# Eighteen operand distances in the second network's first layer: gaps between three weight matrices, each tile's x pieces at a place of its own

## The chip, the cores and the metric

The kernel runs on one core of one Trainium2 chip. The metric is device microseconds of one execution, the median of several; lower is better. Three runs are given for the kernel before. All times below are microseconds (us) unless marked ns.

## The reference

Attention with a decaying state runs over four sequences of 768 tokens, 8 heads of 48 channels. Its 3,072 x 384 result goes through a gated network and then through a second network, the only one that the change touches:

```python
def _moe_ref(x, w_gate, w_val, w_out, rms_g):
    ...
    g = xn @ w_gate
    silu = g * (1.0 / (1.0 + np.exp(-g)))
    val = xn @ w_val
    return (silu * val @ w_out).astype(np.float32)

def _moe2_ref(x, w1, w2, w3, w_out):
    h = np.maximum(np.maximum(x @ w1, x @ w2), x @ w3)
    return (h @ w_out).astype(np.float32)
```

All is float32. In the second network x is 3,072 x 384, w1, w2 and w3 are 384 x 768 and w_out is 768 x 384.

## The kernel before

The tokens are cut into six tiles of 512 (128 tokens of each of the four sequences). Attention of a tile runs interleaved with the gated network of the tile before; a last pass of the gated network runs alone; then the second network goes over the six tiles one after the other. Each engine has its own instruction stream, written out by hand, and the streams meet in semaphores: `after(engine, semaphore, tile, per_tile, nth)` waits for a count.

Every float32 product is made of three matmuls of a rounded type (`split_products`, the lines 484, 485 and 486 of the profile). Each operand is split into a rounded part, hi, and the rest, lo, and the three are hi x hi, hi x lo and lo x hi. In each, a 128 x 128 piece of weights is loaded into TensorE (a LDWEIGHTS record, engine "PEld") and then up to 512 columns of the other operand stream past it (a MATMUL record, engine "PE").

The first layer of the second network, in `phase2_tile` of the tensor block, takes for each of 6 column groups f and each of the matrices n = w1, w2, w3 three chunks c of 128 input channels: 6 x 3 x 3 x 3 = 162 matmuls of 512 columns. The weights stand, x streams. The results go to PSUM banks, ScalarE copies the first of three (line 840), VectorE takes the two maxima (lines 1115 and 1118), ScalarE and GpSimd split the result into hi and lo (lines 857 and 1236). The second layer is 4 x 6 x 3 = 72 matmuls of 384 columns, with the hidden values standing and `wo2` streaming.

x of a tile is loaded from scratch in DRAM to `xf` (the memory of `xn`), and then ScalarE (`split_x2_hi`, line 778) and VectorE (`split_x2_lo`, line 1034) split it into `x_hi` and `x_lo`, three chunks each. They do so for tile i + 1 when the last first-layer matmul of tile i is done, which is while TensorE runs the second layer of tile i. Before the change the buffers are `x_hi` and `x_lo`, which the first network uses too, at the start of the memory that the kernel allocates; `w123` lies behind the first network's weights:

```python
        x_hi = sb("x_hi", [P, KC, TOK], F32R)
        x_lo = sb("x_lo", [P, KC, TOK], F32R)
        xn = sb("xn", [P, B, DM])
        ...
        x1s = sb("x1s", [P, KC, TOK])
        act_h = sb("act_h", [P, 2, TOK])
        ...
        wg = [p1(f"wg_{s}", [P, KC, FF], F32R) for s in ("hi", "lo")]
        wv = [p1(f"wv_{s}", [P, KC, FF], F32R) for s in ("hi", "lo")]
        wo = [p1(f"wo_{s}", [P, FC, DM], F32R) for s in ("hi", "lo")]
        h_hi = p1("h_hi", [P, 2, TOK], F32R)
        h_lo = p1("h_lo", [P, 2, TOK], F32R)
```

P = 128, T = 128, TOK = 512, B = 4, DM = 384, KC = 3, FF = 1536, FC = 12, FF2 = 768, FC2 = 6, TILES = 6; an element has 4 bytes. Buffers are allocated one behind the other, and memory of a closed stage is given out again. On TensorE, tile 0 of the second network is written out and tiles 1 to 5 are a hardware loop (`pe.Fori`); on VectorE and ScalarE tiles 0 and 5 are written out and 1 to 4 are a loop.

Of the kernel before, what the change touches and what calls it, by code (L numbers as in the profile page):

```python
# [31 lines left out]
F32 = mybir.dt.float32  # L32
F32R = mybir.dt.float32r
BF16 = mybir.dt.bfloat16
U8 = mybir.dt.uint8
ACT = mybir.ActivationFunctionType
ALU = mybir.AluOpType
AX = mybir.AxisListType

P = 128  # L40
# [5 lines left out]
def rwkv_moe_kernel(nc, rc, kc, wc, r, k, v, u, g_w1, v_w1, o_w1, rms_g, w1, w2, w3, o_w2, out):  # L46
    B, TILES, _, _, PAIRS, _ = rc.shape
    S, H, D = r.shape[1:]
    DM, FF = g_w1.shape
    FF2 = w1.shape[1]  # L50
    TOK = B * T
    KC = DM // P
# [11 lines left out]
    with ExitStack() as ctx:  # L64
        def sb(name, shape, dt=F32, stack=ctx):
            return stack.enter_context(nc.sbuf_tensor(name, shape, dt))

        def psum(name, shape):
            return ctx.enter_context(nc.psum_tensor(name, shape, F32))

        def sem(name):
            return ctx.enter_context(nc.semaphore(name))
# [5 lines left out]
# [3 lines that stand above are left out]
        xf = xn[:, :, :].rearrange("p b n -> p (b n)").rearrange("p (c t) -> p c t", t=TOK)  # L81
# [36 lines left out]

        late = ExitStack()
        la = lambda name, shape, dt=F32: sb(name, shape, dt, late)  # L120
        w123 = [[la(f"w{i + 1}_{s}", [P, KC, FF2], F32R) for s in ("hi", "lo")] for i in range(3)]
        stage2 = la("stage2", [P, 2, FF2])
        late.close()
        phase1.close()
# [1 line left out]
        p2 = lambda name, shape, dt=F32: sb(name, shape, dt, phase2)  # L126
# [2 lines left out]
        h2_hi = p2("h2_hi", [P, FC2, TOK], F32R)  # L129
        h2_lo = p2("h2_lo", [P, FC2, TOK], F32R)  # L130
        ostage = p2("ostage", [P, 2, DM])
        phase2.close()

        ps_gate = psum("ps_gate", [P, TOK])
        ps_val = psum("ps_val", [P, TOK])
# [68 lines left out]
        x2_hi = sem("x2_hi")  # L204
        x2_lo = sem("x2_lo")
# [11 lines left out]
        def after(eng, s, tile, per_tile=1, nth=0):  # L217

            n = tile * per_tile + nth
            if not isinstance(n, int) or n > 0:  # L220
                eng.wait_ge(s, n)
# [257 lines left out]
        def _(pe):  # L479
            mm = nc.tensor.matmul  # L480

            def split_products(dst, lhs, rhs, start, stop):

                mm(dst, lhs[0], rhs[0], start=start, stop=False)  # L484
                mm(dst, lhs[0], rhs[1], start=False, stop=False)  # L485
                return mm(dst, lhs[1], rhs[0], start=False, stop=stop)  # L486
# [149 lines left out]
            def phase2_tile(i):  # L636
                for f in range(FC2):
                    cols = slice(f * P, (f + 1) * P)
                    for n in range(3):
                        if f == 0:  # L640
                            if isinstance(i, int) and i == 0:
                                pe.wait_ge(wt2_lo, (n + 1) * KC)
                        if isinstance(i, int) and i == 0 and f == 1 and n == 0:
                            pe.wait_ge(x1_copied, KC * PASSES)

                        after(pe, (m1_done, m2_done, m3_done)[n], i, FC2, f - 1)
                        for c in range(KC):
                            if f == 0 and n == 0:
                                after(pe, x2_lo, i, KC, c + 1)
                            wt = w123[n]  # L650
                            last = split_products(bank3[f % 2][n], (wt[0][:, c, cols], wt[1][:, c, cols]),
                                                  (x_hi[:, c, :], x_lo[:, c, :]), c == 0, c == KC - 1)
                        last.then_inc(mm3_done[n], 1)
                if isinstance(i, int) and i == 0:
                    pe.wait_ge(wt2_lo, len(pieces2))

                order = [(b, f) for b in range(B) for f in range(FC2)]
                order.remove((0, FC2 - 1))
                order.insert(FC2 - 1 + FC2 // 2, (0, FC2 - 1))
                for b, f in order:  # L660
                    if f == 0:
                        after(pe, out_copied, i, B, b - 1)
                    after(pe, h2_lo_done, i, FC2, f + 1)
                    toks = slice(b * T, (b + 1) * T)
                    last = split_products(bank_out[b % 2][:, 0:DM], (h2_hi[:, f, toks], h2_lo[:, f, toks]),
                                          (wo2[0][:, f, :], wo2[1][:, f, :]), f == 0, f == FC2 - 1)
                    if f == FC2 - 1:
                        last.then_inc(out_full, 1)


            pe.wait_ge(val_used, FC * PASSES)
            phase2_tile(0)
            with pe.Fori(1, TILES) as i:
                phase2_tile(i)


# [1 line left out]
        def _(act):  # L678
# [92 lines left out]
            def split_x2_hi(i):  # L771
                after(act, xf_in, i, 16, 16)
                if isinstance(i, int) and i == 0:
                    act.wait_ge(val_full, FC * PASSES)
                else:
                    after(act, mm3_done[2], i, FC2, 0)
                for c in range(KC):
                    nc.scalar.activation(x_hi[:, c, :], xf[:, c, :], ACT.Copy).then_inc(x2_hi, 1)

            def load_piece2(n):  # L780
                _, last = loads_before(n)
# [12 lines left out]
            def weight_piece2(n):  # L794
                act.wait_ge(st2_in[stage_of[n]], 16 * (loads_before(n)[0] + 1))
                nc.scalar.activation(pieces2[n][0], stages2[stage_of[n]], ACT.Copy).then_inc(wt2_hi, 1)
                for later in range(4, len(pieces2)):
                    if n == max(later - 3, loads_before(later)[1]):
                        load_piece2(later)
# [34 lines left out]
            def phase2_tile(i, last=False):  # L834
                if isinstance(i, int) and i == 0:
                    act.wait_ge(out_done, FC * PASSES)
                for f in range(FC2):
                    after(act, mm3_done[0], i, FC2, f + 1)
                    after(act, h2_lo_done, i, FC2, f - 1)
                    nc.scalar.activation(h2f[:, f % 2, :], bank3[f % 2][0], ACT.Copy).then_inc(m1_done, 1)  # L840
                    if f:
                        hidden_hi(i, f - 1)
                    if isinstance(i, int) and i == 0 and f % 2 == 0:
                        weight_piece2(EARLY2 + f // 2)
                hidden_hi(i, FC2 - 1)
                if not last:
                    split_x2_hi(i + 1)
                for b in range(B):
                    after(act, out_full, i, B, b + 1)
                    after(act, out_stored[b % 2], i, 16 * B // 2, 16 * (b // 2))  # L850
                    nc.scalar.activation(ostage[:, b % 2, :], bank_out[b % 2][:, 0:DM], ACT.Copy
                                         ).then_inc(out_copied, 1)

            def hidden_hi(i, f):
                after(act, m3_done, i, FC2, f + 1)
                after(act, out_full, i, B, 0)
                nc.scalar.activation(h2_hi[:, f, :], h2f[:, f % 2, :], ACT.Copy).then_inc(h2_hi_done, 1)  # L857

            phase2_tile(0)
            with act.Fori(1, TILES - 1) as i:  # L860
                phase2_tile(i)
            phase2_tile(TILES - 1, last=True)


        @block.vector
        def _(dve):
            tt = nc.vector.tensor_tensor
# [163 lines left out]
            def split_x2_lo(i):  # L1031
                for c in range(KC):
                    after(dve, x2_hi, i, KC, c + 1)
                    tt(x_lo[:, c, :], xf[:, c, :], x_hi[:, c, :].bitcast(F32), ALU.subtract).then_inc(x2_lo, 1)

            def x_split_lo(n):
                toks = tokens(n)[0]
# [72 lines left out]
            def phase2_tile(i, last=False):  # L1110
                for f in range(FC2):
                    dst = h2f[:, f % 2, :]
                    after(dve, m1_done, i, FC2, f + 1)
                    after(dve, mm3_done[1], i, FC2, f + 1)
                    tt(dst, dst, bank3[f % 2][1], ALU.max).then_inc(m2_done, 1)  # L1115
                    after(dve, m2_done, i, FC2, f + 1)
                    after(dve, mm3_done[2], i, FC2, f + 1)
                    tt(dst, dst, bank3[f % 2][2], ALU.max).then_inc(m3_done, 1)
                    if isinstance(i, int) and i == 0 and f % 2 == 0:
                        weight_piece2(EARLY2 + f // 2)  # L1120
                if not last:
                    split_x2_lo(i + 1)

            phase2_tile(0)
            with dve.Fori(1, TILES - 1) as i:
                phase2_tile(i)
            phase2_tile(TILES - 1, last=True)


        @block.gpsimd  # L1130
# [147 lines left out]
```

## Time and profile before

| | us |
|---|---|
| median of three runs | 1040.18 |
| lowest and highest | 1038.83, 1042.09 |
| the profiled execution | 1042.37 |
| its span, first to last instruction | 1040.6 |
| TensorE busy with matmuls in it | 997.7 |
| from the first matmul of the second network to the end | 298.55 |

A profile is one execution. An engine's busy time is the time in which it had at least one record running. Neighbouring matmuls overlap in the records: each has a duration of 0.33 to 0.40 us, while one starts every 0.17 to 0.24 us. So the pace is read from starts, not from durations. Starts are printed to 10 ns; a pace is therefore taken over many matmuls, from the first start to the last.

### The profile page before, as it was taken

To read this page: it belongs to the slowest core of one execution; us is meant where nothing else is said; L and a number is where in the kernel's file an instruction comes from. 1 tells how busy PE (TensorE), PEld (TensorE's weight loads), DVE (VectorE), ACT (ScalarE), POOL (GpSimd) and SP (SyncE) were. 2 spreads that over 40 slices of the span, in tenths; PEclk is the share of its full clock that TensorE was granted. 3 is DMA by queue.
4 is the path that set the end of the run, shared out by engine and by line. 5 is a ranking of instruction groups with operands and counts; after the bars stand their busy time and mean duration, and the time that the engine had idled before them with its cause. 6 is when DMAs were issued, how large, how long until landed. Compare 5 with 4: busy or idle time off the path is not lost.

```text
span 1040.6 us, 16737 instructions
## 1 busy us (share of the span) xinstructions
PE 997.7 (96%) x5680; PEld 882.3 (85%) x5680; DVE 623.3 (60%) x1047; ACT 246.2 (24%) x488; POOL 489.2 (47%) x540
## 2 busy tenths in 40 slices
PE   4778988899999999999999999999999999999998
PEld 4778988888888888888888888888888888888988
DVE  7878798988776877778776867444332212121221
ACT  2132312222123121222122212333322212121211
POOL 7656586857574757566674757212010201011111
PEclk9689999999999999999999999999999999999999
DMA  6533312212112120303021220201301010101000
GB/s 200 161 89 96 97 46 77 74 50 96 58 60 63 55 97 3 108 12 133 18 88 34 91 63 5 92 31 61 122 0 61 1 61 8 53 15 45 23 8 31
DMA packets 36221, 64.65 MB, mean 62 GB/s; under 512 B 4928, under 2 KB 22720, under 8 KB 36160
## 3 DMA queue, kind: packets, MB, share of 16 engines
q1 hardware_dynamic: 30288, 52.12, 15.2%
q10 hardware_dynamic: 5872, 11.80, 3.5%
q8 instruction: 28, 0.46, 0.2%
q14 instruction: 33, 0.27, 0.1%
HBM read 54.46 MB, written 9.44 MB: 61 GB/s over the span
## 4 chain that ended last, share of the span: by engine, by line
PE 84%; DVE 5%; POOL 5%; issue 3%; ACT 1%; DMA 0%; SPq 0%; ACTq 0%; POOLq 0%; DVEq 0%
PE ps_sc L503 10%; PE ps_acc L484 8%; PE ps_acc L486 8%; PE ps_acc L485 8%; PE ps_gate L484 6%; PE ps_gate L486 6%; PE ps_val L484 6%; PE ps_gate L485 6%; PE ps_val L486 5%; PE ps_val L485 5%; PE ps_desk L527 3%; PE ps_sc L486 2%; PE ps_sc L484 2%; PE ps_sc L485 2%; POOL kT L1168 2%
## 5 line engine op out<-in xcount | busy, mean ns | idle before, releaser
L503 PEld LDWEIGHTS ps_sc<-rB,kT 128*128 128x128 f32 x1152 | 155.8, 202 | 36.8 <-DVE rB L913 18.0
L503 PE MATMUL ps_sc<-rB,kT 128*128 128x128 f32 x1152 | 162.2, 288 | 25.8 <-DVE A L938 10.6
L1168 POOL TENSOR_TENSOR kT<-kT,wT 128x256 f32<-128x256 f32 x164 | 140.0, 853 | 83.9 <-PE ps_sc L503 56.4
L1236 POOL TENSOR_TENSOR h_lo<-h2f,h_hi 128x512 fp32r<-128x512 f32 x36 | 46.3, 1285 | 247.5 <-ACT h_hi L857 247.5
L1139 POOL TENSOR_TENSOR h_lo<-act_h,h_hi 128x512 fp32r<-128x512 f32 (+1 forms) x83 | 97.7, 1178 | 108.8 <-ACT h_hi L707 104.2
L1175 POOL TENSOR_TENSOR rB<-rB,wT 64x256 f32<-64x256 f32 x144 | 121.1, 841 | 11.3
L913 DVE TENSOR_TENSOR rB<-rB,wT 64x256 f32<-64x256 f32 x144 | 96.1, 672 | 30.4 <-PE ps_sc L503 23.7
L484 PE MATMUL ps_gate<-x_hi,wg_hi 128*128 128x512 f32 (+1 forms) x252 | 97.0, 385 | 8.9 <-DVE act_h L888 6.9
L707 ACT ACTIVATE h_hi<-act_h 128x512 fp32r<-128x512 f32 (+1 forms) x84 | 47.9, 571 | 230.4 <-DVE act_h L891 230.2
L938 DVE COPY_PREDICATED A<-mask,ps_sc 128x512 f32<-128x512 uint8 x120 | 98.9, 824 | 0.0
L484 PE MATMUL ps_acc<-h_hi,wo_hi 128*128 128x512 f32 (+1 forms) x252 | 95.7, 380 | 0.5 <-POOL h_lo L1139 0.3
L484 PE MATMUL ps_val<-x_hi,wv_hi 128*128 128x512 f32 (+1 forms) x252 | 96.2, 382 | 0.0
L703 ACT ACTIVATE act_h<-ps_gate 128x512 f32<-128x512 f32 (+1 forms) x84 | 45.1, 536 | 212.8 <-PE ps_gate L486 212.6
L486 PE MATMUL ps_gate<-x_hi,wg_lo 128*128 128x512 f32 (+1 forms) x252 | 91.8, 364 | 0.0
L486 PE MATMUL ps_val<-x_hi,wv_lo 128*128 128x512 f32 (+1 forms) x252 | 91.7, 364 | 0.0
L485 PE MATMUL ps_gate<-x_lo,wg_hi 128*128 128x512 f32 (+1 forms) x252 | 91.2, 362 | 0.0
L485 PE MATMUL ps_val<-x_lo,wv_hi 128*128 128x512 f32 (+1 forms) x252 | 91.1, 362 | 0.0
L925 DVE TENSOR_TENSOR wT<-wT 128x128 f32<-128x128 f32 (+6 forms) x160 | 77.1, 490 | 23.4 <-POOL rB L1175 21.5
L486 PE MATMUL ps_acc<-h_hi,wo_lo 128*128 128x512 f32 (+1 forms) x252 | 90.9, 361 | 0.0
L485 PE MATMUL ps_acc<-h_lo,wo_hi 128*128 128x512 f32 (+1 forms) x252 | 90.5, 359 | 0.0
L1115 DVE TENSOR_TENSOR h2f<-h2f,ps_val 128x512 f32<-128x512 f32 x18 | 12.4, 688 | 106.2 <-PE ps_val L486 106.2
L891 DVE TENSOR_TENSOR act_h<-act_h,ps_val 128x512 f32<-128x512 f32 (+1 forms) x84 | 51.4, 612 | 35.4 <-PE ps_val L486 34.1
(136 smaller groups left out, 2028.7 us busy)
## 6 DMA issues: line engine op xcount, KB each, us to landing
kT<-in_k_channels SPq DMA_DIRECT2D x24, 256.0 KB, 3.4
wT<-in_w_channels SPq DMA_DIRECT2D x24, 256.0 KB, 4.0
rB<-in_r_channels SPq DMA_DIRECT2D x48, 128.0 KB, 2.6
kL<-in_k_tokens SPq DMA_DIRECT2D x24, 192.0 KB, 2.4
rL<-in_r_tokens SPq DMA_DIRECT2D x24, 192.0 KB, 2.5
vL<-in_v_tokens SPq DMA_DIRECT2D x24, 192.0 KB, 2.4
x_scratch<-x1s SPq DMA_DIRECT2D x6, 768.0 KB, 4.4
xn<-x_scratch SPq DMA_DIRECT2D x6, 768.0 KB, 4.3
```

The costliest lines, as they stand in the source:

```text
L484: mm(dst, lhs[0], rhs[0], start=start, stop=False)
L485: mm(dst, lhs[0], rhs[1], start=False, stop=False)
L486: return mm(dst, lhs[1], rhs[0], start=False, stop=stop)
L503: last = mm(ps_sc[:, j, q * T:(q + 1) * T], kT[2 * duo + j][:, q, :], rights, start=True, stop=True)
L707: nc.scalar.activation(h_hi[:, f % 2, toks], act_h[:, f % 2, toks], ACT.Copy).then_inc(h_hi_done, 1)
L891: tt(hidden, hidden, ps_val[:, toks], ALU.mult).then_inc(val_used, 1)
L913: tt(new, old, block_decay(2 * duo + j, 1 << level, 0, HEAD_ROWS[0]), ALU.mult).then_inc(r_even_scaled, 1)
L925: tt(left, left, half(w[:, :, :], h, 1)[:, :, 0:1], ALU.mult).then_inc(tot_done, 1)
L938: nc.vector.copy_predicated(dst, every_head.broadcast_to([P, H, n, h]), src.rearrange("p (g n h) -> p g n h", g=H, h=h)).then_inc(scores_u ...
L1139: tt(h_lo[:, f % 2, toks], act_h[:, f % 2, toks], h_hi[:, f % 2, toks].bitcast(F32), ALU.subtract).then_inc(h_lo_done, 1)
L1168: tt(half(kT[b][:, :, :], h, 0), half(kT[b][:, :, :], h, 0), block_decay(b, h, 1), ALU.mult).then_inc(k_scaled, 1)
L1175: tt(new, old, block_decay(b, h, 0, HEAD_ROWS[1]), ALU.mult).then_inc(r_odd_scaled, 1)
```

## The change

Three things are changed. Between w1 and w2, and between w2 and w3, unused gaps of 16 and 32 elements (64 and 128 bytes) are allocated. The split x of the second network no longer goes to `x_hi` and `x_lo` but to four new rooms (hi and lo, for even and for odd tiles), which lie in memory that the first network's weights no longer need, and in its room each tile's x starts at an offset of its own, `X2_AT`, counted in elements: 0, 4, 8, 12, 2, 6. As these offsets are numbers of the program, the loops over the second network's tiles on TensorE, ScalarE and VectorE are written out. GpSimd's and SyncE's streams stay as they are, and no semaphore count changes.

```diff
@@ -118,7 +118,11 @@
-        w123 = [[la(f"w{i + 1}_{s}", [P, KC, FF2], F32R) for s in ("hi", "lo")] for i in range(3)]
+        w123 = []
+        for i, gap in enumerate((0, 16, 32)):
+            if gap:
+                la(f"gap{i}", [P, gap])
+            w123.append([la(f"w{i + 1}_{s}", [P, KC, FF2], F32R) for s in ("hi", "lo")])
@@ -129,7 +133,15 @@
         ostage = p2("ostage", [P, 2, DM])
+        x2_room = [[p2(f"x2_{s}{i}", [P, KC * TOK + P], F32R) for s in ("hi", "lo")] for i in range(2)]
         phase2.close()
+
+        X2_AT = (0, 4, 8, 12, 2, 6)
+
+        def x2_piece(i, lo):
+
+            room = x2_room[i % 2][lo]
+            return room[:, X2_AT[i]:X2_AT[i] + KC * TOK].rearrange("p (c t) -> p c t", t=TOK)
...
@@ -649,9 +661,9 @@
                             wt = w123[n]
                             last = split_products(bank3[f % 2][n], (wt[0][:, c, cols], wt[1][:, c, cols]),
-                                                  (x_hi[:, c, :], x_lo[:, c, :]), c == 0, c == KC - 1)
+                                                  (x2_piece(i, 0)[:, c, :], x2_piece(i, 1)[:, c, :]), c == 0, c == KC - 1)
                         last.then_inc(mm3_done[n], 1)
...
@@ -669,8 +681,7 @@
             pe.wait_ge(val_used, FC * PASSES)
-            phase2_tile(0)
-            with pe.Fori(1, TILES) as i:
+            for i in range(TILES):
                 phase2_tile(i)
@@ -775,7 +786,7 @@
                 for c in range(KC):
-                    nc.scalar.activation(x_hi[:, c, :], xf[:, c, :], ACT.Copy).then_inc(x2_hi, 1)
+                    nc.scalar.activation(x2_piece(i, 0)[:, c, :], xf[:, c, :], ACT.Copy).then_inc(x2_hi, 1)
@@ -1031,7 +1040,7 @@
                     after(dve, x2_hi, i, KC, c + 1)
-                    tt(x_lo[:, c, :], xf[:, c, :], x_hi[:, c, :].bitcast(F32), ALU.subtract).then_inc(x2_lo, 1)
+                    tt(x2_piece(i, 1)[:, c, :], xf[:, c, :], x2_piece(i, 0)[:, c, :].bitcast(F32), ALU.subtract).then_inc(x2_lo, 1)
@@ -1121,10 +1130,8 @@
-            phase2_tile(0)
-            with dve.Fori(1, TILES - 1) as i:
-                phase2_tile(i)
-            phase2_tile(TILES - 1, last=True)
+            for i in range(TILES):
+                phase2_tile(i, last=i == TILES - 1)
```

The same is done to ScalarE's loop, and some tests of the tile number are shortened.

In the rows below, `x2_hi1` is the hi room of the odd tiles. First TensorE's stream where tile 0 of the second network ends and tile 1 begins, before:

```order
L484 MATMUL ps_desk<-wo2_hi,h2_hi 128x384
L485 MATMUL ps_desk<-wo2_lo,h2_hi 128x384
L486 MATMUL ps_desk<-wo2_hi,h2_lo 128x384
L673 UNCONDITIONAL_BRANCH
L673 ISA
L221 ISA
L484 MATMUL ps_gate<-x_hi,w1_hi 128x512
L485 MATMUL ps_gate<-x_lo,w1_hi 128x512
L486 MATMUL ps_gate<-x_hi,w1_lo 128x512
L221 REGISTER_ALU
L484 MATMUL ps_gate<-x_hi,w1_hi 128x512
```

And after, at the same place:

```order
L496 MATMUL ps_desk<-wo2_hi,h2_hi 128x384
L497 MATMUL ps_desk<-wo2_lo,h2_hi 128x384
L498 MATMUL ps_desk<-wo2_hi,h2_lo 128x384
L496 MATMUL ps_gate<-x2_hi1,w1_hi 128x512
L497 MATMUL ps_gate<-x2_lo1,w1_hi 128x512
L498 MATMUL ps_gate<-x2_hi1,w1_lo 128x512
```

The matmuls stand in the same order; the branch and the register instructions between them are gone, and x comes from another buffer. VectorE's stream at the end of tile 1, inside its loop, before:

```order
L1115 TENSOR_TENSOR h2f<-h2f,ps_acc 128x512
L1118 TENSOR_TENSOR h2f<-h2f,ps_acc 128x512
L221 ISA
L1034 TENSOR_TENSOR x_lo<-xn,x_hi 128x512
L221 REGISTER_ALU
L1034 TENSOR_TENSOR x_lo<-xn,x_hi 128x512
```

And after, at the end of tile 1:

```order
L1124 TENSOR_TENSOR h2f<-h2f,ps_acc 128x512
L1127 TENSOR_TENSOR h2f<-h2f,ps_acc 128x512
L1043 TENSOR_TENSOR x2_lo0<-xn,x2_hi0 128x512 x3
```

The three subtractions that make lo stay where they were, behind the tile's last maximum, and write to the even tiles' room.

## Rows read from the trace of the kernel before

**Rows 1.** the page: span, and each engine's busy time, share, instructions.
```profile
span 1040.6 us, 16737 instructions
PE 997.7 (96%) x5680; PEld 882.3 (85%) x5680; DVE 623.3 (60%) x1047; ACT 246.2 (24%) x488; POOL 489.2 (47%) x540
```

**Rows 2.** the page, the chain that ended last, by engine.
```profile
PE 84%; DVE 5%; POOL 5%; issue 3%; ACT 1%; DMA 0%; SPq 0%; ACTq 0%; POOLq 0%; DVEq 0%
```

**Rows 3.** windows, the second network's tiles 0, 1 and 4.
```profile
core 0: us, PE busy (x) PEld busy (x) DVE busy (x) ACT busy (x) POOL busy (x), PEclk, DMA share, GB/s
742.05:791.28 49.23, 49.23 (x235) 42.91 (x234) 13.44 (x18) 13.63 (x24) 7.74 (x6) 1.00 0.15 53
791.28:840.55 49.27, 49.27 (x236) 42.91 (x235) 10.83 (x15) 10.35 (x19) 7.71 (x6) 1.00 0.09 33
939.08:988.35 49.27, 49.27 (x236) 42.91 (x235) 10.83 (x15) 10.35 (x19) 7.71 (x6) 1.00 0.10 32
```

**Rows 4.** timeline, TensorE's matmuls, tile 0: start, duration in us.
```profile
742.05 0.39 PE L484 MATMUL ps_gate<-x_hi,w_hi 128*128 128x512 f32 x1
744.10 0.39 PE L484 MATMUL ps_val<-x_hi,w_hi 128*128 128x512 f32 x1
...
778.55 0.39 PE L486 MATMUL ps_acc<-x_hi,w_lo 128*128 128x512 f32 x1
```

**Rows 5.** timeline, TensorE's matmuls, second layer of tile 0.
```profile
785.74 0.33 PE L485 MATMUL ps_sc<-wo_lo,h_hi 128*128 128x384 f32 x1
...
791.11 0.33 PE L486 MATMUL ps_desk<-wo_hi,h_lo 128*128 128x384 f32 x1
```

**Rows 6.** timeline, TensorE's weight loads, start of tile 0.
```profile
742.05 0.19 PEld L485 LDWEIGHTS ps_gate<-x_lo,w_hi 128*128 128x128 f32 x1
742.29 0.19 PEld L486 LDWEIGHTS ps_gate<-x_hi,w_lo 128*128 128x128 f32 x1
```

**Rows 7.** timeline, TensorE's matmuls, start of tile 1.
```profile
791.28 0.39 PE L484 MATMUL ps_gate<-x_hi,w_hi 128*128 128x512 f32 x1
791.51 0.40 PE L485 MATMUL ps_gate<-x_lo,w_hi 128*128 128x512 f32 x1
791.74 0.40 PE L486 MATMUL ps_gate<-x_hi,w_lo 128*128 128x512 f32 x1
791.98 0.39 PE L484 MATMUL ps_gate<-x_hi,w_hi 128*128 128x512 f32 x1
...
793.36 0.39 PE L484 MATMUL ps_val<-x_hi,w_hi 128*128 128x512 f32 x1
```

**Rows 8.** groups by line, attention's matmuls, 98 to 660 us.
```profile
L503 PE MATMUL ps_sc<-rB,kT 128*128 128x128 f32 x984 | 129.8, 275 | 7.6 <-DVE A L938 6.0 <-issue 1.2 <-POOL rB L1175 0.3
L527 PE MATMUL ps_desk<-vL,A 128*128 128x48 f32 x352 | 42.0, 272 | 0.0
L522 PE MATMUL ps_desk<-state,rD 128*128 128x96 f32 x160 | 21.0, 274 | 0.1
```

**Rows 9.** timeline, attention scores of level 1, then of level 2.
```profile
175.95 1.07 PE L503 MATMUL ps_sc<-rB,kT 128*128 128x128 f32 x8
...
226.68 1.05 PE L503 MATMUL ps_sc<-rB,kT 128*128 128x128 f32 x8
```

**Rows 10.** the page, DMA queues: packets, MB, share of 16 engines.
```profile
q8 instruction: 28, 0.46, 0.2%
```

**Rows 11.** timeline, ScalarE's and VectorE's x pieces, tiles 0 and 1.
```profile
738.99 1.66 ACT L778 ACTIVATE x_hi<-xn 128x512 fp32r<-128x512 f32 x3
739.73 1.89 DVE L1034 TENSOR_TENSOR x_lo<-xn,x_hi 128x512 fp32r<-128x512 f32 x3
...
780.30 1.66 ACT L778 ACTIVATE x_hi<-xn 128x512 fp32r<-128x512 f32 x3
780.95 2.57 DVE L1034 TENSOR_TENSOR x_lo<-xn,x_hi 128x512 fp32r<-128x512 f32 x3 [1.22 <-ACT x_hi L778]
```

More of the change, by code:

```diff
@@ L640, in phase2_tile @@
                         if f == 0:
-                            if isinstance(i, int) and i == 0:
+                            if i == 0:
                                 pe.wait_ge(wt2_lo, (n + 1) * KC)
-                        if isinstance(i, int) and i == 0 and f == 1 and n == 0:
+                        if i == 0 and f == 1 and n == 0:
                             pe.wait_ge(x1_copied, KC * PASSES)
@@ L651, in phase2_tile @@
                             last = split_products(bank3[f % 2][n], (wt[0][:, c, cols], wt[1][:, c, cols]),
-                                                  (x_hi[:, c, :], x_lo[:, c, :]), c == 0, c == KC - 1)
+                                                  (x2_piece(i, 0)[:, c, :], x2_piece(i, 1)[:, c, :]), c == 0, c == KC - 1)
                         last.then_inc(mm3_done[n], 1)
-                if isinstance(i, int) and i == 0:
+                if i == 0:
                     pe.wait_ge(wt2_lo, len(pieces2))
@@ L857, in hidden_hi @@
                 nc.scalar.activation(h2_hi[:, f, :], h2f[:, f % 2, :], ACT.Copy).then_inc(h2_hi_done, 1)
-            phase2_tile(0)
-            with act.Fori(1, TILES - 1) as i:
-                phase2_tile(i)
-            phase2_tile(TILES - 1, last=True)
+            for i in range(TILES):
+                phase2_tile(i, last=i == TILES - 1)
         @block.vector
@@ L1122, in phase2_tile @@
                     split_x2_lo(i + 1)
-            phase2_tile(0)
-            with dve.Fori(1, TILES - 1) as i:
-                phase2_tile(i)
-            phase2_tile(TILES - 1, last=True)
+            for i in range(TILES):
+                phase2_tile(i, last=i == TILES - 1)
         @block.gpsimd
```

## The prediction

> **What bounds the kernel now.** I read the page first: the span and how much of it TensorE computes [rows 1]. TensorE is busy 96% of the span, and the chain that ended last is 84% TensorE [rows 2]. So a term counts if it changes the pace of the matmuls or makes them wait. The change touches only the second network, so I then cut that part into its six tiles (three of them in [rows 3]). The reader is to see that in each of the first five tiles TensorE is busy for the whole 49.23 to 49.27 us, that the clock is at its upper level (1.00, 2.4 GHz), and that VectorE, ScalarE and GpSimd are busy for 7.7 to 13.6 us of it. Nothing there waits for data; only the number of matmuls and their pace count.
>
> The pace stands in the timeline. In tile 0 the first layer has 162 matmuls of 512 columns. The first starts at 742.05, the last at 778.55 [rows 4], so 161 gaps take 36.50 us: 226.7 ns each. In the second layer, 384 columns, the rows at 785.74 and 791.11 are 31 gaps apart [rows 5]: 173.2 ns each. The two paces differ by 53.5 ns for 128 columns, 0.418 ns a column. 512 columns at that rate take 214 ns, so about 13 ns of each gap are not columns. Those 13 ns are the only thing here that a change of addresses could win: 972 first-layer matmuls (162 in each of 6 tiles).
>
> What can addresses do to them? The weight load of the next matmul starts with the current one [rows 4, 6]: the matmul at 742.05 streams x while the load at 742.05, 0.19 us long, reads the next 128 columns of weights. Both read SBUF at the same time. How far apart they read follows from the declarations. From x_hi to w1_hi lie four buffers of 6,144 bytes per partition, act_h with 4,096, six weight matrices of 18,432 and two h buffers of 4,096: 147,456 bytes, 288 times 512. Each further matrix is 9,216 bytes (18 times 512), each x chunk 2,048, each c step of the weights 3,072, each f step 512. So before the change every first-layer pair is at a distance that is a whole multiple of 512 bytes.
>
> **The change part by part.**
> Distances. The gaps shift w2 by 64 bytes and w3 by 64 + 128 = 192. The x pieces shift by 0, 16, 32, 48, 8 and 24 bytes, tile by tile. Modulo 256 this gives 6 x 3 = 18 different distances, and only tile 0 with w1 (54 matmuls) keeps the old one; 918 matmuls move. No row shows a first-layer matmul at another distance. From both sides: at best the 13.3 ns vanish, 918 x 13.3 ns = 12.2 us. At worst every gap is as long as the longest that the trace has between unstalled 512-column matmuls, 0.24 us at the start of tile 1 [rows 7]: 13.3 ns more, 12.2 us the other way. I take zero, for two reasons. Distances already differ between c, f, hi and lo by several multiples of 512, and the gap does not move. And both streams walk: the 128 weight columns are 512 bytes, x is 2,048 bytes in one matmul, so if both take their columns evenly over their records' time the distance between the two reading points sweeps through hundreds of bytes within each matmul. A shift of the start by 8 to 192 bytes then only changes where the sweep begins. The attention stage is weak support: moving operands whose starts step by 192 bytes (vL for A) and 384 bytes (state for rD) have records of 272 and 274 ns, against 275 ns for rB, which is always on the 512-byte grid [rows 8]. Weak, since these are short matmuls of two operand shapes and the weight load paces them.
>
> What speaks against zero: the gap isn't a constant of the operation. The first nine matmuls of tile 1 take 791.28 to 793.36, 2.08 us, those of tile 0 742.05 to 744.10, 2.05 us [rows 4, 7], and the first three gaps in tile 1 are 0.23, 0.23 and 0.24 us where the steady ones are 0.2267. The operands and distances are the same in both tiles; so a stall of some nanoseconds inside a matmul depends on how the two streams stand in time. That is why I keep over four in ten for a real effect.
>
> The Trainium skill, page "TensorE: Matmul & The Clock Gate", section "Part 2: What happens when you issue a matmul", says that TensorE has two independent SBUF read ports and that loading the next weights takes nothing from the running matmul. By this rule the change is worth exactly zero. The same page (section "Wait — 56ns, not 53.3ns?") gives 215.7 ns for 512 columns; the trace has 226.7, so 11 ns of each gap are something that the page does not have. An estimate from that page: if the new distances removed them, 918 x 11 = 10.1 us.
>
> Starts inside a 16-byte group. Tiles 4 and 5 start at 8 and 24 bytes. The nearest row is attention level 1, where rB is read in runs of two values, 8 bytes: eight records take 1.07 us, with longer runs 1.05 [rows 9]: 2.5 ns for 128 columns. Four times that, 10 ns, for 324 matmuls is 3.2 us. That is an upper bound, since a contiguous row only adds a partial group at its start; I take zero.
>
> Unrolled loops. TensorE, ScalarE and VectorE lose a branch and register arithmetic at each tile. TensorE pays 2.08 against 2.05 us at a tile start: 0.03 us x 5 = 0.15 us, if the loop is the reason and not the step from 384 to 512 columns; I take 0.15. The longer program must be fetched: instruction queue 8 takes 0.2% of the DMA engines' time now [rows 10], and tile 0, which is written out straight already, runs 49.23 us against 49.27 in the loop [rows 3]. Zero.
>
> ScalarE's and VectorE's x pieces. They write as many values as before, to other places, and no wait moves: the next tile's x is still split only after all first-layer matmuls of this one, so two rooms bring no earlier start. Their cover: in tile 0 ScalarE splits from 780.30 and VectorE ends at 780.95 + 2.57 = 783.52 [rows 11]; the next tile needs it at 791.28, 7.8 us later. At the border between the networks the cover is thin: VectorE's three pieces run from 739.73 to 741.62, the first is needed at 742.05 and the third some 1.4 us later [rows 4, 11]. Pieces twice as long would end at 743.51, and the first (0.63 us now) would be ready at 740.99: at most 0.1 to 0.2 us of waiting, once. What is queued behind them on VectorE is tile 0's first maximum, which is due only after 18 matmuls of the tile, 4.1 us past 742.05. Zero.
>
> Sum: -0.15 us on a span of 1040.6. The profiled execution took 1042.37 us, the median of the three runs is 1040.18; I put the difference on the median: 1040.0.
>
> **The rivals.**
> 1. The distance has no effect (above): 1040.0, own range 1038.5 to 1041.5. For it: the constant gap over all multiples of 512, the walking streams. Against it: the gaps that vary by nanoseconds. Chance 0.56.
> 2. Faster: equal remainders are the bad case, because the weight read and the x read meet in the same place of SBUF, and other distances part them. For it: 13 ns per matmul, whether 384 or 512 columns stream, which is what a fixed number of meetings with a fixed 128-column load would cost. All shifted pairs free: 1040.0 - 12.2 = 1028. More likely some distances help and others don't: half gives 6.1 us, 1034. Chance 0.24.
> 3. Slower: the old remainder is the good case, and a shifted pair stalls all the time as at the start of tile 1. There nine gaps average 231.1 ns, 4.4 more: 918 x 4.4 ns = 4.1 us, 1044. It decides from 3.4 ns per shifted matmul (3.1 us, 0.3%); bound 1052. Against it: nothing marks the old place as special. Chance 0.13.
> 4. Slower: the starts at 8 and 24 bytes cost 10 ns each, in tiles 4 and 5 alone: 3.2 us, 1043. Against it: a row has one partial group in 128. Chance 0.07.
>
> **How the numbers follow.** A difference of 0.3%, 3.1 us, is about what a measurement of this kernel can tell from no change. Same: case 1, 0.56. Faster: case 2, 0.24. Slower: cases 3 and 4, 0.20. The predicted time is case 1's. The range runs from 1033, case 2 with half of its bound and a little more, to 1046, cases 3 and 4 with their own sizes and some more. It leaves out case 2 near its full bound (about 0.10) and case 3 near its bound (about 0.06).
>
> **What would show it.** Right: in the changed profile all six tiles take 49.2 us, and the first layer's gap is 226.7 ns in each tile and for each matrix. Case 2 or 3 would show as 18 different paces, by tile and by matrix, with tile 0 and w1 at 226.7. Case 4 would show as tiles 4 and 5 longer by 1.6 us each, tiles 1 to 3 unchanged. VectorE's split in the changed tiles longer than 2.57 us would show that writes at odd places cost, hidden. The prediction is wrong if any steady gap is not 226.7.

## The result, and the profile after

The change makes the kernel slower: 1046.20 us against 1040.87, medians of six runs each, ratio 1.0054 (95% interval 1.0041 to 1.0068). I had forecast 1040.0 and a range from 1033 to 1046.

The page and the timeline of the changed kernel, span and engines first, then the first matmul of the second network's tiles 1 to 5, the first of tile 2's second layer (877.88) and the last of all (start, duration in us):

```profile
span 1044.2 us, 16568 instructions
PE 999.0 (96%) x5680; PEld 879.3 (84%) x5680; DVE 622.8 (60%) x1047; ACT 246.2 (24%) x488; POOL 490.4 (47%) x540
...
790.09 0.39 PE L496 MATMUL ps_gate<-x_hi,w_hi 128*128 128x512 f32 x1
...
840.09 0.39 PE L496 MATMUL ps_gate<-x_hi,w_hi 128*128 128x512 f32 x1
...
877.88 0.33 PE L496 MATMUL ps_sc<-wo_hi,h_hi 128*128 128x384 f32 x1
...
890.38 0.39 PE L496 MATMUL ps_gate<-x_hi,w_hi 128*128 128x512 f32 x1
...
940.66 0.39 PE L496 MATMUL ps_gate<-x_hi,w_hi 128*128 128x512 f32 x1
...
990.87 0.39 PE L496 MATMUL ps_gate<-x_hi,w_hi 128*128 128x512 f32 x1
...
1040.96 0.34 PE L498 MATMUL ps_desk<-wo_hi,h_lo 128*128 128x384 f32 x1
```

The second network begins at 740.33 (next fence) and ends with the span at 1044.2: 303.87 us, against 298.55 before, 5.3 more. That is as much as the medians differ (5.33). The two profiled spans differ by less, 3.6 us, because this execution reached the second network 1.7 us earlier (740.33 against 742.05; in all the traces of this case it is 739.4 to 744.7); the change touches nothing in the part before but where w2 and w3 lie. TensorE is still never idle in the second network up to its last matmul, and the granted clock there is 1.00, as before. The tiles take 49.76, 50.00, 50.29, 50.28 and 50.21 us, where [rows 3] has 49.23 to 49.27. So each tile is longer, tile 0 least.

The same number of matmuls runs at another pace. The nine-matmul groups of tile 0, first the one of w1, then w2, w3 and w1 again (timeline, the first matmul of each group):

```profile
740.33 0.39 PE L496 MATMUL ps_gate<-x_hi,w_hi 128*128 128x512 f32 x1
...
742.37 0.40 PE L496 MATMUL ps_val<-x_hi,w_hi 128*128 128x512 f32 x1
...
744.47 0.39 PE L496 MATMUL ps_sc<-x_hi,w_hi 128*128 128x512 f32 x1
...
746.53 0.39 PE L496 MATMUL ps_acc<-x_hi,w_hi 128*128 128x512 f32 x1
...
748.59 0.40 PE L496 MATMUL ps_acc<-x_hi,w_hi 128*128 128x512 f32 x1
```

w1, the only one at the old distance, takes 2.04 us for nine, as before. w2 (-64 bytes) takes 2.10, w3 (-192) 2.06: 233 and 229 ns each for 226.7. w1 after w3 takes 2.06 too (2.05 in the later groups), so a group at the old distance does not start at its old pace right away. Tile 2, whose x is 32 bytes on, has no group at the old pace: from 840.09 to its second layer at 877.88 are 162 matmuls in 37.79 us, 233.3 ns each. Over the six tiles the first layer has 5.35 us more (225.87 against 220.52), 5.8 ns for each of the 918 moved matmuls. Averaged over its six groups, each of the eighteen pairs of tile and matrix lies between 227.6 ns (tile 0, w1) and 234.6 ns (tile 3, w2). The second layer, whose operands kept their distances, takes 12.3 us as before.

VectorE's split, for which I had left a margin, did not change (timeline, x_lo for tile 1; [rows 11] has 2.57 too):

```profile
779.78 2.57 DVE L1043 TENSOR_TENSOR x_lo<-xn,x_hi 128x512 fp32r<-128x512 f32 x3 [1.22 <-ACT x_hi L789]
```

### The profile page after: what moved, and what is told of

Same layout as the page of the kernel before. It is cut to its first block, busy times and chain, and to the rows that moved or that the text cites. A ratio compares the mean times of both kernels' runs of the same rounds, so it can differ in the third digit from the quotient of the medians.

```text
span 1044.2 us, 16568 instructions
## 1 busy us (share of the span) xinstructions
PE 999.0 (96%) x5680; PEld 879.3 (84%) x5680; DVE 622.8 (60%) x1047; ACT 246.2 (24%) x488; POOL 490.4 (47%) x540
## 4 chain that ended last, share of the span: by engine, by line
PE 83%; DVE 6%; POOL 5%; issue 3%; ACT 1%; DMA 0%; SPq 0%; ACTq 0%; POOLq 0%; DVEq 0%
PE ps_sc L515 9%; PE ps_acc L496 8%; PE ps_acc L498 8%; PE ps_acc L497 8%; PE ps_gate L496 6%; PE ps_gate L498 6%; PE ps_val L496 5%; PE ps_gate L497 5%; PE ps_val L498 5%; PE ps_val L497 5%; PE ps_desk L539 3%; PE ps_sc L497 2%; PE ps_sc L498 2%; PE ps_sc L496 2%; POOL kT L1175 2%
## 5 line engine op out<-in xcount | busy, mean ns | idle before, releaser
L515 PE MATMUL ps_sc<-rB,kT 128*128 128x128 f32 x1152 | 159.7, 285 | 27.2 <-POOL rB L1182 12.9
L515 PEld LDWEIGHTS ps_sc<-rB,kT 128*128 128x128 f32 x1152 | 153.5, 199 | 38.1 <-DVE rB L922 19.4
L718 ACT ACTIVATE h_hi<-act_h 128x512 fp32r<-128x512 f32 (+1 forms) x84 | 47.9, 571 | 229.0 <-DVE act_h L900 228.8
```

Of the source, the lines that this page charges most:

```text
L515: last = mm(ps_sc[:, j, q * T:(q + 1) * T], kT[2 * duo + j][:, q, :], rights, start=True, stop=True)
L718: nc.scalar.activation(h_hi[:, f % 2, toks], act_h[:, f % 2, toks], ACT.Copy).then_inc(h_hi_done, 1)
```

## The experiments

Distance below is the remainder of (address of x less address of the weights) modulo 256 bytes. Paces are first start to first start of the next stretch over the number of matmuls. All experiments are variants of the changed kernel or of the one before; ratios are against the kernel before on the same chip, with the 95% interval in brackets, and the us behind a ratio are its distance from 1 times the median of before.

### Undo the distances, keep the rest

```diff
-        for i, gap in enumerate((0, 16, 32)):
+        for i, gap in enumerate((0, 0, 0)):
-        X2_AT = (0, 4, 8, 12, 2, 6)
+        X2_AT = (0, 0, 0, 0, 0, 0)
```

> The changed kernel with both kinds of offsets at zero: no gaps between the matrices, every tile's x at the start of its room. The new rooms and the written-out tiles stay. If the distances cost the time, all six tiles are back at 49.2 us and the median lies at that of before, within 1 us. If the rooms or the written-out loops cost it, the tiles stay at 49.8 to 50.3 us and the time 5 us above before.

Ratio 1.0001 (0.9988 to 1.0014). The first matmuls of tiles 0, 1, 2 and of tile 1's second matrix (timeline):

```profile
741.03 0.39 PE L496 MATMUL ps_gate<-x_hi,w_hi 128*128 128x512 f32 x1
...
790.26 0.39 PE L496 MATMUL ps_gate<-x_hi,w_hi 128*128 128x512 f32 x1
...
792.34 0.39 PE L496 MATMUL ps_val<-x_hi,w_hi 128*128 128x512 f32 x1
...
839.52 0.39 PE L496 MATMUL ps_gate<-x_hi,w_hi 128*128 128x512 f32 x1
```

Tiles of 49.23 and 49.26 us: the new rooms and the written-out loops cost nothing. They gain nothing either. Tile 1's first nine matmuls still take 2.08 us (790.26 to 792.34) though there is no loop any more, so my 0.15 us for the branches was wrong. That the slower start comes from the step from 384 to 512 columns, the other cause that I had named, is not shown either: in a run below one tile is entered from 384 columns without it, and one has it without such a step.

### The gaps alone, and the x offsets alone

The two halves of the change, each with the other set to zero as above.

> The gaps alone (w2 64 bytes on, w3 192), x of all tiles at the start of its room. By distances every tile is as tile 0 of the changed kernel: w1 about 227.6 ns, w2 232.9, w3 229.6 a matmul, first layer 37.27 us, a tile 49.75: 6 x 0.52 = 3.1 us over before. If only x's offsets mattered: as before.

> The x offsets alone, no gaps: in a tile all three matrices are at the same distance (0, 16, 32, 48, 8, 24 bytes). If the distance itself costs, w1, w2 and w3 of a tile all have w1's pace in the changed kernel (about 231.4, 234.1, 233.5, 232.4, 233.8 ns in tiles 1 to 5): some 5 us over before. If a change of distance from one matrix to the next costs, and a constant one settles, tiles 1 to 5 run at 226.7 ns and the time is that of before.

Gaps alone: ratio 1.0027 (1.0014 to 1.0040), 2.8 us. Offsets alone: 1.0048 (1.0031 to 1.0066), 5.0 us. Tiles 1 and 2 with the gaps alone, then with the offsets alone tiles 0 to 4 and tile 4's first matmul of 384 columns (timeline, first matmuls):

```profile
789.73 0.39 PE L496 MATMUL ps_gate<-x_hi,w_hi 128*128 128x512 f32 x1
...
839.52 0.39 PE L496 MATMUL ps_gate<-x_hi,w_hi 128*128 128x512 f32 x1
```

```profile
740.24 0.39 PE L496 MATMUL ps_gate<-x_hi,w_hi 128*128 128x512 f32 x1
...
789.46 0.39 PE L496 MATMUL ps_gate<-x_hi,w_hi 128*128 128x512 f32 x1
...
839.47 0.39 PE L496 MATMUL ps_gate<-x_hi,w_hi 128*128 128x512 f32 x1
...
889.75 0.39 PE L496 MATMUL ps_gate<-x_hi,w_hi 128*128 128x512 f32 x1
...
940.03 0.39 PE L496 MATMUL ps_gate<-x_hi,w_hi 128*128 128x512 f32 x1
...
977.82 0.34 PE L496 MATMUL ps_sc<-wo_hi,h_hi 128*128 128x384 f32 x1
```

With the gaps alone tile 1 takes 49.79 us, and so do tiles 2 to 4 (tile 0, 49.75). With the offsets alone tile 0 is back at 49.22 us, and tiles 1 and 2 take 50.01 and 50.28; in tile 4 the 162 matmuls run from 940.03 to 977.82, 233.3 ns each. There all three matrices are at one distance, 8 bytes, for 162 matmuls on end and the pace does not recover. So it is the distance that costs, not a change of distance. The two halves do not add up to the whole (2.8 + 5.0 against 5.3), as the combined distances are others, and none that is made of both shifts costs the sum of the two: the slowest, tile 3 with w2, is 7.9 ns over 226.7, where its halves are 6.6 and 6.2.

### Both operands moved together, and larger distances

```diff
-        for i, gap in enumerate((0, 16, 32)):
+        for i, gap in enumerate((16, 0, 0)):
-        X2_AT = (0, 4, 8, 12, 2, 6)
+        X2_AT = (16, 0, 32, 80, 112, 48)
```

> A gap of 64 bytes ahead of w1 and none later; x of the six tiles 64, 0, 128, 320, 448 and 192 bytes into its room. So tile 0 has both operands 64 bytes on, at distance 0; tiles 1 to 5 have x less w at -64, +64, +256, +384 and +128 bytes, the same for all three matrices. By distance tile 0 runs at 226.7 ns and tile 1 near 232.9 (w2 of tile 0 in the changed kernel). If an operand's own address counts, tile 0 is slower. If only changes of distance count, all are at 226.7. A multiple of 256 bytes may be as good as 0; then tile 3 is at 226.7.

Ratio 1.0027 (1.0014 to 1.0040). First matmul and first second-layer matmul (384 columns) of tiles 0, 1, 2 and 3; in tiles 0 and 3 also the tenth matmul (`ps_val`):

```profile
741.92 0.39 PE L496 MATMUL ps_gate<-x_hi,w_hi 128*128 128x512 f32 x1
...
743.99 0.39 PE L496 MATMUL ps_val<-x_hi,w_hi 128*128 128x512 f32 x1
...
778.68 0.34 PE L496 MATMUL ps_sc<-wo_hi,h_hi 128*128 128x384 f32 x1
...
791.18 0.39 PE L496 MATMUL ps_gate<-x_hi,w_hi 128*128 128x512 f32 x1
...
828.99 0.34 PE L496 MATMUL ps_sc<-wo_hi,h_hi 128*128 128x384 f32 x1
...
841.49 0.40 PE L496 MATMUL ps_gate<-x_hi,w_hi 128*128 128x512 f32 x1
...
878.58 0.33 PE L496 MATMUL ps_sc<-wo_hi,h_hi 128*128 128x384 f32 x1
...
891.07 0.39 PE L496 MATMUL ps_gate<-x_hi,w_hi 128*128 128x512 f32 x1
...
893.11 0.39 PE L496 MATMUL ps_val<-x_hi,w_hi 128*128 128x512 f32 x1
...
927.78 0.34 PE L496 MATMUL ps_sc<-wo_hi,h_hi 128*128 128x384 f32 x1
```

| tile | distance, bytes | first layer, us | a matmul, ns |
|---|---|---|---|
| 0 | 0, both 64 on | 36.8 | 226.9 |
| 1 | -64 | 37.8 | 233.3 |
| 2 | +64 | 37.1 | 229.0 |
| 3 | +256 | 36.7 | 226.7 |
| 4, 5 | +128 | 37.6 | 232.4 |

Moving both operands by 64 bytes leaves the steady pace as it was (the 0.2 ns of tile 0 are its first nine matmuls), moving one does not, and 256 bytes are as good as zero. (Tiles 4 and 5 had +384 and +128, the same modulo 256, and ran at the same pace.) The sign matters: +64 costs 2.2 ns, -64 costs 6.7.

The same trace speaks on the slow start. Tile 3 is entered from the 384-column layer, and its first nine matmuls take 2.04 us. Tile 0 is entered from the first network's 512-column matmuls and takes 2.07. So neither the loop nor the step in columns is the whole of it, and what sets the start of a tile stays open.

### Six more distances, and the second layer

X offsets of 1, 36, 40, 44, 63 and 62 elements, no gaps between the matrices, and

```diff
+        p2("gap_h2", [P, 16])
         h2f = p2("h2f", [P, 2, TOK])
         ...
+        p2("gap_back", [P, 48])
```

> Six more distances, the same for the three matrices of a tile: x is 4, 144, 160, 176, 252 and 248 bytes on (modulo 256: 4, -112, -96, -80, -4, -8). No theory says which of them is good; so far 0 and 256 give 226.7 ns and all others 228.9 to 234.1. If only the multiples of 256 are good, none is at 226.7 or under. Also, the hidden values h2, which stand in the second layer, lie 64 bytes on, so that wo2 less h2 is -64 bytes there: if the law holds at 384 columns too, that layer's gap goes from 173.3 to 180.0 ns (as 226.7 goes to 233.3), 6 x 72 x 6.7 ns = 2.9 us in all; if it is special to the first layer, it stays at 173.3.

Ratio 1.0087 (1.0065 to 1.0108), the slowest of all. The first layers take 38.47, 37.79, 37.94, 37.79, 37.20 and 37.78 us: 237.5 ns a matmul at +4 bytes, 233.3 at 144, 176 and 248, 234.2 at 160, 229.6 at 252. With those above, fourteen distances other than 0 have had a tile of their own, and all are slower than 0. The second layer surprised (first and last of its 72 matmuls, tiles 0 and 1):

```profile
779.90 0.34 PE L498 MATMUL ps_sc<-wo_hi,h_hi 128*128 128x384 f32 x1
...
792.20 0.34 PE L500 MATMUL ps_desk<-wo_hi,h_lo 128*128 128x384 f32 x1
...
830.17 0.34 PE L498 MATMUL ps_sc<-wo_hi,h_hi 128*128 128x384 f32 x1
...
842.71 0.33 PE L500 MATMUL ps_desk<-wo_hi,h_lo 128*128 128x384 f32 x1
```

71 gaps take 12.30 us in tile 0 and 12.54 in tile 1: 173.3 and 176.7 ns, at one and the same distance. Tiles 3 and 5 are at 176.7 too, tiles 2 and 4 at 174.7. The three tiles at 176.7 are those whose first layer ran at 233.3 ns; they are also the three odd ones. The last pair of experiments below asks which of the two it is.

### Which two reads must agree

```diff
+            hi = la(f"w{i + 1}_hi", [P, KC, FF2], F32R)
+            la(f"gap{i}_lo", [P, 16])
+            lo = la(f"w{i + 1}_lo", [P, KC, FF2], F32R)
+            w123.append([hi, lo])
+            la(f"gap{i}_back", [P, 48])
-        X2_AT = (0, 4, 8, 12, 2, 6)
+        X2_AT = ((0, 16), (0, 0), (16, 16), (16, 0), (0, 4), (0, 32))
```

Each pair is the offset of x_hi and of x_lo in a tile, in elements.

> Which two reads count. All three w_lo lie 64 bytes on, w_hi on the old place; x_hi and x_lo have offsets of their own. In tile 0 x_lo is 64 bytes on and x_hi is not. Then every matmul streams x from the same remainder as the weights that are loaded meanwhile for the next matmul, but in the second and third matmul of each three x and its own weights differ by 64. If the load that overlaps is what counts, tile 0 runs at 226.7 ns; if a matmul's own weights count, it is at 229 or more. Tile 1 has both x at 0: the load of w_lo overlaps x_lo at -64, one in three. Tile 2 has both x 64 on: two of three at +64. Tile 3 has x_hi alone 64 on: +64, -64, +64. Tile 4: 0, -48, 0; tile 5: 0, +64, 0.

One run, 1045.65 us. Tile 0, first matmul and first of its second layer:

```profile
741.64 0.39 PE L498 MATMUL ps_gate<-x_hi,w_hi 128*128 128x512 f32 x1
...
779.07 0.34 PE L498 MATMUL ps_sc<-wo_hi,h_hi 128*128 128x384 f32 x1
```

37.43 us, 231.0 ns. My idea that only the stream and the load beside it must agree gives 226.7 and falls. The other idea, a matmul's own weights, asked for 229 or more and is not refuted by this tile, but the prices of the table don't add up by it either: 0, +64 and -64 would average 229.6. Tiles 1, 3, 4 and 5, whose distances have no pattern in common, are all at 231.1 or 231.2; tile 2 is at 229.1. The counterpart leaves all weights alone (the gaps are zero) and moves x_lo only, but for tile 5:

```diff
-        X2_AT = (0, 4, 8, 12, 2, 6)
+        X2_AT = ((0, 64), (0, 16), (0, 32), (0, 48), (0, 4), (16, 32))
```

> All weights at the old place, x_hi at 0 in tiles 0 to 4, x_lo on by 256, 64, 128, 192 and 16 bytes; in tile 5 x_hi 64 and x_lo 128. If each pair of a stream and the load beside it has its own price and these add up, one in three pays: tile 0 226.7 ns, tile 1 226.7 + 2.2/3 = 227.4, tile 3 226.7 + 6.7/3 = 228.9, tile 2 about 228.6, tile 4 about 228.4. If what costs is that neighbouring streams start at different remainders, all of tiles 1 to 4 are near 231.1 ns, as four tiles of the run with w_lo 64 bytes on were, and tile 0 at 226.7.

One run, 1044.68 us. Tiles 2 and 3, first matmul and first of the second layer:

```profile
840.04 0.39 PE L496 MATMUL ps_gate<-x_hi,w_hi 128*128 128x512 f32 x1
...
877.84 0.34 PE L496 MATMUL ps_sc<-wo_hi,h_hi 128*128 128x384 f32 x1
...
890.35 0.39 PE L496 MATMUL ps_gate<-x_hi,w_hi 128*128 128x512 f32 x1
...
927.42 0.33 PE L496 MATMUL ps_sc<-wo_hi,h_hi 128*128 128x384 f32 x1
```

x_lo on by 256 (tile 0): 226.7 ns. By 192 (tile 3): 37.07 us, 228.9 ns, which is what adding up one -64 in three gives. By 64 (tile 1) 231.9, by 128 (tile 2) 233.3, by 16 (tile 4) 232.0: neither of the two theories. (Tile 5, x_hi on by 64 and x_lo by 128, is at 231.2.) So prices of single pairs don't add up, and a change from one stream to the next does not have one price. Which pairs of reads disturb each other stays open.

### Fewer weight columns

```diff
-        for i, gap in enumerate((0, 16, 32)):
+        for i, gap in enumerate((0, 0, 0)):
+        W_COLS = (128, 96, 64, 32, 128, 64)
-        X2_AT = (0, 4, 8, 12, 2, 6)
+        X2_AT = (0, 0, 0, 0, 48, 48)
-                    cols = slice(f * P, (f + 1) * P)
+                    cols = slice(f * P, f * P + W_COLS[i])
```

> What the 13.3 ns over the 213.3 ns of 512 columns are. Tiles 0 to 3 have distance 0 and load 128, 96, 64 and 32 weight columns a matmul (the other hidden channels of these tiles are left out); tiles 4 and 5 have distance -64 and load 128 and 64. If each group of weight columns read takes a slot from the stream of x, the excess falls with the columns: 226.7, about 223, 220, 217 ns; and at distance -64 from 233.3 to about 223 for 64 columns. If it is a fixed price of a change of weights, all of tiles 0 to 3 stay at 226.7 and tiles 4 and 5 at 233.3.

One run, 1048.75 us. Tile 3 (32 columns): a weight load, then first matmul and first of the second layer:

```profile
899.96 0.11 PEld L499 LDWEIGHTS ps_acc<-x_hi,w_lo 128*32 128x32 f32 x1
```

```profile
893.47 0.40 PE L497 MATMUL ps_gate<-x_hi,w_hi 128*32 128x512 f32 x1
...
931.00 0.34 PE L497 MATMUL ps_sc<-wo_hi,h_hi 128*128 128x384 f32 x1
```

The loads are shorter, 0.11 us for 0.19, and the matmuls are not: 37.53 us, 231.7 ns each; 230.0 with 96 and with 64 columns; at distance -64 232.7 with 64 columns for 233.3. Both theories fall, the second only by 3 to 5 ns at distance 0. The 13 ns are no price per weight column, and they are no constant: at distance 0 a full load of 128 columns is the best of the four.

### The first network and attention

In the kernel before, 64 bytes ahead of the gate weights (and 192 ahead of the output weights, which keep their remainder):

```diff
+        p1("gap_g", [P, 16])
         wg = [p1(f"wg_{s}", [P, KC, FF], F32R) for s in ("hi", "lo")]
         wv = [p1(f"wv_{s}", [P, KC, FF], F32R) for s in ("hi", "lo")]
+        p1("gap_back", [P, 48])
```

> The kernel before, with the first network's gate and value weights 64 bytes on (the output weights and all behind them on the old remainder), so x less weights is -64 bytes in 1512 matmuls of the first network. Nothing else is changed. If the law of the second network's first layer holds here, they take 233.3 ns each for 226.7: 10.1 us in all, of which the last pass (216 of them, nothing beside them) must show 1.4 us, and the interleaved passes most of theirs, since TensorE is busy over 90% there: +6 to +10 us. If the effect is special to the second network, the time stays.

Ratio 1.0054 (1.0035 to 1.0073), 5.6 us. A gate group, a value group and an output group of nine in the last pass (first matmul of each and of the next):

```profile
690.93 0.40 PE L486 MATMUL ps_gate<-x_hi,wg_hi 128*128 128x512 f32 x1
...
693.04 0.39 PE L486 MATMUL ps_val<-x_hi,wv_hi 128*128 128x512 f32 x1
...
695.13 0.39 PE L486 MATMUL ps_acc<-h_hi,wo_hi 128*128 128x512 f32 x1
...
697.20 0.40 PE L486 MATMUL ps_gate<-x_hi,wg_hi 128*128 128x512 f32 x1
```

Gate and value groups take 2.10 and 2.09 us, 233 ns a matmul, as in the second network. The output group, whose operands are at distance 0, takes 2.07 us: it begins slow and recovers in its course. From the last of attention's score matmuls (648.1 in both) to the second network are 95.5 us against 93.9: +1.6, where I expected 1.4. The price of -64 bytes is the same in another stage. Of the interleaved passes I expected up to 8.7 us more; the ratio leaves about 4 for them, give or take 2. Where the two profiled executions reach the end of these passes doesn't tell (the last score matmul stands at 648.1 in both, and at 645.5 in the attention experiment below), but the pace in them does. Over some 700 gaps under 0.26 us behind a gate or value matmul the mean is 229.8 ns in the trace of before and 233.2 here. So these matmuls, which attention's keep interrupting, were 3 ns slower than 226.7 to begin with and had only 3.4 ns to lose, half of my 6.7.

The same in attention, whose matmuls have 128 columns (a fourth gap behind the last kT brings the rest back):

```diff
+            if b:
+                at_(f"gap_k{b}", [P, 16])
             kT.append(at_(f"kT{b}", [P, PAIRS, T]))
```

> The kernel before, with the four kT buffers of attention 0, 64, 128 and 192 bytes on (64-byte gaps between them), so rB less kT is 0, -64, -128 and -192 bytes for the four sequences. These matmuls have 128 columns, and the weight load paces them (111 ns a record). If only a stream of x that is longer than the load is slowed by distance, the pace stays 111 ns for all four and the time is that of before. If the two reads disturb each other whatever the sizes, the sequences 1 to 3 are slower, by up to 6.7 ns a record; 3/4 of 1152 records, at most 5.8 us. A distance that is better than 0 here would make the kernel faster.

Ratio 0.9990 (0.9976 to 1.0004): the same. The group of these matmuls between 95 and 650 us (count | busy, mean ns of one) has records of 275 ns, as in [rows 8]:

```profile
L508 PE MATMUL ps_sc<-rB,kT 128*128 128x128 f32 x984 | 129.8, 275 | 7.7 <-DVE A L943 6.1 <-issue 1.3 <-POOL rB L1180 0.3
```

A duration is no pace, but the starts say the same: within the groups of eight that nothing interrupts, the four sequences start a record every 111.5, 111.4, 111.8 and 111.5 ns here and every 111.6, 111.4, 111.5 and 111.6 ns before. Two things keep this from being a test of the number of columns alone. These matmuls take plain float32 operands, not the rounded type, and each of them shows as two records. And `rights`, the part of rB that is read, begins h values into a row, h = 2, 4, ... 64 by level: 8 to 256 bytes. So my 0, -64, -128 and -192 bytes were wrong; they hold only where h is 64, and the kernel before had several distances here already. Levels 2 to 6 are all at 111.0 to 111.2 ns before, level 1 at 113.6.

### The second layer alone, entered always alike

`gap_h2` of 16 and then of 48 elements in the kernel before, with 48 and then 16 behind h2 so that what follows keeps its remainder; nothing else.

> The kernel before, its first layer untouched at distance 0 (226.7 ns), with the hidden values h2 alone 64 bytes on: wo2 less h2 is -64 bytes in the second layer. In the run that had this beside six x offsets the layer ran at 173.3 ns in tile 0, 176.7 in tiles 1, 3 and 5, 174.7 in tiles 2 and 4, at one and the same distance. If the pace of a stretch hangs on how it is entered, here, where every tile is entered from the same steady pace, all six tiles must have the same pace. If it hangs on the tile's number or its data, the pattern 173.3, 176.7, 174.7 comes back.

> The same with h2 192 bytes on: wo2 less h2 is +64 modulo 256. If +64 costs 2.2 ns a matmul at 384 columns as it does at 512, the second layer is at 175.5 ns in all tiles (+1 us in all); at -64 the like would be 180.0. If shorter matmuls have a table of prices of their own, the order of the two can be another.

One run each: 1040.96 and 1042.85 us, beside 1041.61. First and last second-layer matmul, tile 1 with 16 elements and then with 48:

```profile
826.28 0.34 PE L486 MATMUL ps_sc<-wo_hi,h_hi 128*128 128x384 f32 x1
...
838.68 0.34 PE L488 MATMUL ps_desk<-wo_hi,h_lo 128*128 128x384 f32 x1
```

```profile
828.65 0.34 PE L486 MATMUL ps_sc<-wo_hi,h_hi 128*128 128x384 f32 x1
...
840.96 0.34 PE L488 MATMUL ps_desk<-wo_hi,h_lo 128*128 128x384 f32 x1
```

At -64 bytes all six tiles take 12.40 us, 174.7 ns; the three different paces of the run above are gone, the odd tiles' 176.7 with them. That is as expected if the pace of a stretch depends on how it is entered; it was tried with one way of entering only, so it is not shown. At +64 all are at 173.3 to 173.4 ns, no slower than at distance 0. So prices at 384 columns are others than at 512 (1.3 and 0 ns instead of 6.7 and 2.2), and neither of my two numbers, 180.0 and 175.5, was right.

## Why the prediction was wrong

**The step that failed** is the first term of the sum: "I take zero" for the distances. It measured +5.35 us, and the offsets set back to zero gave the time of before. I gave two reasons. That the pace is constant over all multiples of 512 bytes is true, but it says nothing about other remainders: with a period of 256 bytes every one of them is the same distance. The trace of before had no first-layer matmul at any other. The second was that both reads walk, so that a shift of the start only moves the beginning of the sweep. Its conclusion is refuted: 4 bytes cost 10.8 ns a matmul. The support from attention was weaker than I said. I had taken rB to be read always on the 512-byte grid, and it is read from 8 to 256 bytes into a row; and a shift of kT showed no effect there, whether because of the plain float32 type, the 128 columns, or because the load and not the stream sets the pace. None of these was tried alone.

**The row that pointed the right way** was the one against zero. [rows 7] against [rows 4] showed the same matmuls at the same distances at two paces. It carried rival 3, to which I gave 0.13: "the old remainder is the good case". Its size was 4.4 ns for each of 918 matmuls, 4.1 us; measured were 5.8 ns, 5.35 us. That the sizes are this close is luck in part: nothing shows that a shifted pair stalls as the start of tile 1 does, and single distances cost from 2.2 to 10.8 ns. My objection, that nothing marks the old place as special, was wrong: at 512 columns it is the best of all tried. Rival 2, which I held for nearly twice as likely, would have needed a distance better than zero.

**Right**: the bound (all of the change in time is the matmuls' pace), the second layer unchanged (173.4 to 173.7 ns), the fetch of the longer program at no cost, the x pieces hidden, the clock at its upper level. **Rival 4**, a price for starts inside 16 bytes, is refuted by tiles 4 and 5, no slower than 2 and 3, and by the run with the offsets alone: 8 bytes run at 233.3 ns, as 32 and 48 bytes do, and 24 bytes at 234.0. **The unrolled loops** were mis-sized, 0.15 us where the runs show none.

The rule of the Trainium skill (page "TensorE: Matmul & The Clock Gate", section "Part 2: What happens when you issue a matmul"), that loading the next weights takes nothing from the running matmul, had made such a shift free. The runs disagree with that: 4 bytes between the two add 10.8 ns a matmul, and the measurement decides. Whether the two reads get in each other's way, or something else makes the distance count, no run shows.

**What stays open** is the mechanism. Shown are: the relation of the two addresses counts and not the place of both together (one common shift of 64 bytes tried), its period is 256 bytes where that was tried (256 itself, 384 against 128), 0 is the best of the fifteen distances tried for 512-column matmuls, the effect exists in both networks, it is smaller at 384 columns for the two distances tried, and attention's 128-column float32 matmuls don't show it. Not explained are the 13 ns that remain at distance 0, why one distance had three paces at 384 columns, what makes a tile start slowly, and which pairs of reads disturb each other. No version here beats the kernel before beyond the uncertainty.

## What to carry to other kernels

Where long matmuls with a new weight load each run back to back, try streamed and stationary operands at starts that are equal modulo 256 bytes, and mind buffers of odd size allocated between them: shifts of 4 to 192 bytes cost 1 to 5% of the pace here, with 512 columns of the rounded type. Read the pace as first start to last start over many matmuls, and compare what stages leave over columns divided by the clock: here 13.3 ns at distance 0, with 512 columns and with 384, and 20.0 at -64 bytes with 512. And a constant in a trace is evidence only for the values that the kernel visited: all of the first layer's were the same one.

## What the runs showed of the hardware

- First-layer pace by distance, 512 columns, 128 weight columns: 0 and 256 bytes 226.7 ns; +64 229; -4 229.6; +16 231.6; 128 232.4; +8, +32, +48, -8, -64, -80, -112 233.3; +24 234.0; -96 234.2; +4 237.5. The smallest shift forward costs the most, and its mirror image, -4, little. Most of these come from one tile of one execution each, so whether they too depend on how a tile is entered is not known; -64 was at 233.3 in two runs.
- Some paces fit one step: 226.7, 233.3 and 173.3 ns are 34, 35 and 26 times 6.67 ns (16 periods of 2.4 GHz); 228.9 and 231.1 are 34 1/3 and 34 2/3, and single gaps then go up and down between 0.22 and 0.24 us. Others (229.6, 232.4, 237.5, 174.7) don't fit. That a stream falls into step with something is a guess from the numbers.
- A stretch at distance 0 behind one at another distance starts slower: after w3 at +64, w1 in the gaps-alone run takes 2.05 us for nine, and after value groups at -64 the output group 2.07, for 2.04.
- The same distance at 384 columns, -64 bytes, ran at 173.3, 174.7 and 176.7 ns within one execution, each pace constant over a tile.
